# Masked attention and two MLP layers on one core: where q is split, how maxima are taken, the mask's place in a score tile, and single x operations per head

## What is computed

```python
scores = scale * np.matmul(q, k.transpose(0, 1, 3, 2))      # scale = 1/8
mask = block_i >= block_j                                   # blocks of 64 tokens
scores = np.where(mask, scores, -1000000000.0)
scores = scores - np.max(scores, axis=-1, keepdims=True)
attn = np.exp(scores)
attn = attn / (np.sum(attn, axis=-1, keepdims=True) + 1e-09)
attn_out = np.matmul(attn, v)
x = attn_out.transpose(0, 2, 1, 3).reshape(2304, 512)
h = x @ w_in;  x = (h * np.clip(h + 3.0, 0.0, 6.0) / 6.0) @ w_out      # first layer, 512 -> 2048 -> 512
h = x @ w_in2; out = (h * np.tanh(softplus(h))) @ w_out2               # second layer
```

## Time and profile before

| | |
|---|---|
| median of 3 runs | 995.29 us (994.14 to 995.41) |
| the profiled execution's own time | 994.92 us |
| its span | 993.1 us |
| PE busy | 963.6 us, 97% of the span |
| DVE busy | 759.8 us, 77% |
| ACT busy | 648.4 us, 65% |
| POOL busy | 464.0 us, 47%, all of it in the first 512 us |
| granted TensorE clock | 1.00 throughout |

### The profile page before, as it was taken

One profiled execution on the slowest core, in us unless ns is written; L12 is line 12 of the kernel. 1 busy time (PEld: TensorE's weight loads), 2 busy tenths in 40 slices (PEclk: granted clock), 3 DMA queues, 4 the chain that ended last, 5 costly groups with the idle time before them and its releaser, 6 DMA issues.

```text
span 993.1 us, 17891 instructions
## 1 busy us (share of the span) xinstructions
PE 963.6 (97%) x6132; PEld 858.2 (86%) x6132; DVE 759.8 (77%) x1283; ACT 648.4 (65%) x1429; POOL 464.0 (47%) x441
## 2 busy tenths in 40 slices
PE   6999999999999999999999999999999999999998
PEld 5887888899888888998889999899899898998996
DVE  5998888878686866879797786876877877776654
ACT  6888888856555554544445556777777777776663
POOL 7888899967676576968686680000000000000000
PEclk9999999999999999999999999999999999999999
DMA  6778867564689978587977545546645645465255
GB/s 160 211 189 228 222 167 200 151 172 147 221 286 318 321 257 288 182 290 274 316 245 256 199 153 188 222 158 229 219 170 205 230 178 194 170 232 195 93 186 197
DMA packets 81914, 211.49 MB, mean 213 GB/s; under 512 B 12320, under 2 KB 19104, under 8 KB 81824
## 3 DMA queue, kind: packets, MB, share of 16 engines
q1 hardware_dynamic: 81744, 210.06, 65.0%
q10 hardware_dynamic: 80, 0.29, 0.1%
HBM read 170.39 MB, written 39.92 MB: 212 GB/s over the span
## 4 chain that ended last, share of the span: by engine, by line
PE 87%; DVE 7%; issue 3%; ACT 2%; DMA 1%; POOL 1%; SPq 0%; ACTq 0%; DVEq 0%; POOLq 0%
PE psum L956 36%; PE psum L839 11%; PE psum L840 11%; PE psum L841 11%; PE psum L789 5%; PE psum L768 5%; PE psum L744 3%; PE psum L749 3%; DVE ebuf L1519 1%; DVE glo L1525 1%; DMA ext_d<-ext_made 1%; DVE wlo L1417 1%; PE psum L747 1%; DVE ext_made L1425 1%; DMA qkin<-in_qk 1%
## 5 line engine op out<-in xcount | busy, mean ns | idle before, releaser
L956 PE MATMUL psum<-ghi,osplit 128*128 128x512 f32 (+1 forms) x640 | 215.3, 370 | 0.3 <-POOL osplit L1770 0.3
L839 PE MATMUL psum<-xhi,whi 128*128 128x256 f32 (+1 forms) x640 | 187.6, 293 | 2.0 <-ACT snap L1166 2.0
L841 PE MATMUL psum<-xhi,wlo 128*128 128x256 f32 (+1 forms) x640 | 187.5, 293 | 0.0
L840 PE MATMUL psum<-xlo,whi 128*128 128x256 f32 (+1 forms) x640 | 187.4, 293 | 0.0
L956 PE MATMUL psum<-osplit,ghi 128*128 128x512 f32 x576 | 181.2, 396 | 1.4 <-DVE glo L1525 1.4
L1525 DVE SCALAR_TENSOR_TENSOR glo<-ebuf,ghi 128x512 fp32r<-128x512 f32 x144 | 129.9, 902 | 22.5 <-ACT ghi L1214 14.2
L839 PEld LDWEIGHTS psum<-xhi,whi 128*128 128x128 f32 x640 | 121.4, 190 | 15.0 <-ACT snap L1166 3.2
L1770 POOL TENSOR_TENSOR osplit<-oraw,osplit 128x512 fp32r<-128x512 f32 x80 | 117.5, 1471 | 35.7 <-ACT osplit L1133 31.7
L956 PEld LDWEIGHTS psum<-ghi,osplit 128*128 128x128 f32 x640 | 118.1, 189 | 15.8 <-issue 0.4
L840 PEld LDWEIGHTS psum<-xlo,whi 128*128 128x128 f32 x640 | 121.2, 189 | 10.1
L1214 ACT ACTIVATE ghi<-ebuf 128x512 fp32r<-128x512 f32 x144 | 90.1, 626 | 59.4 <-DVE ebuf L1519 37.4
(11 more groups left out here) (113 smaller groups left out, 2252.2 us busy)
## 6 DMA issues: line engine op xcount, KB each, us to landing
ext<-ext_d SPq DMA_DIRECT2D x56, 768.0 KB, 4.4
osplit<-o_d SPq DMA_DIRECT2D x80, 512.0 KB, 5.2
oraw<-in_w_out SPq DMA_DIRECT2D x80, 256.0 KB, 5.8
qkin<-in_qk SPq DMA_DIRECT2D x63, 288.0 KB, 4.3
wraw<-in_w_in SPq DMA_DIRECT2D x32, 512.0 KB, 5.3
ext_d<-ext_made SPq DMA_DIRECT2D x32, 384.0 KB, 5.8
attn_t<-ostage SPq DMA_DIRECT2D x64, 144.0 KB, 3.1
o_d<-staged SPq DMA_DIRECT2D x32, 256.0 KB, 5.4
```

Source lines behind the costliest of these rows:

```text
L839: pe.matmul(dst, hi, xh, start=(start and cc == 0), stop=False, skip_group_check=True)
L840: pe.matmul(dst, hi, xl, start=False, stop=False, skip_group_check=True)
L841: last = pe.matmul(dst, lo, xh, start=False, stop=(stop and cc == 1), skip_group_check=True)
L956: last = pe.matmul(bank(Y_BANK + c, n), stat, mov, start=(first and m == 0), stop=(final and m == 2), skip_group_check=True)
```

## The change

Five edits, all in attention.

1. q is no longer scaled. ScalarE writes `qs` high directly (`split_q_hi`, now L1024), for all heads; GpSimd's cast of q (L1648) is gone. Since `qs` of head n+1 must be free, ScalarE now waits for the scores of head n+1, and the operation stands before the exponential of tile 3 instead of behind that of tile 0.
2. The factor 1/8 goes into the exponential's scale and into the maximum. The maximum is now a `tensor_scalar` (times -1/8) that writes the scaled tile into `prob`, with an accumulator output by minimum into `negmax`.
3. The mask is float32r and is the first matmul of a tile (start=True); `khi` follows. The constants are made with two more GpSimd casts at the start.
4. GpSimd's order: `khi`, v low, x, `klo`, `qs` low.
5. x of the first block: the addition in steps 12, 14, 16 and 18, the multiplication in steps 13, 15, 17 and 19, the rest one step earlier; its four loads go in pairs in steps 9 and 10.

```diff
-EARLY_X_LOAD, NEXT_X_LOAD = (9, 10, 11, 12), (27, 29)
-EARLY_X_ADD, EARLY_X_MIX, EARLY_X_HI, EARLY_X_LO = (14, 16, 18, 20), 21, (22, 23, 24), (23, 24, 25)
+EARLY_X_LOAD, NEXT_X_LOAD = {9: (0, 1), 10: (2, 3)}, (27, 29)
+EARLY_X_ADD, EARLY_X_SCALE, EARLY_X_MIX = (12, 14, 16, 18), (13, 15, 17, 19), 20
+EARLY_X_HI, EARLY_X_LO = (21, 22, 23), (22, 23, 24)
...
-        mask_rows = sb("mask_rows", [P, P], BF16)
-        mask_val = sb("mask_val", [P, DH], BF16)
-        negmax = [sb(f"negmax{s}", [P, NT], F32) for s in range(2)]
+        mask_rows = sb("mask_rows", [P, P], F32R)
+        mask_val = sb("mask_val", [P, DH], F32R)
...
                 for pb, k0, w in pieces:
-                    pe.matmul(bank(pb, w), q_tile, khi[s][:, k0:k0 + w], start=True, stop=False)
                     if i < 4:
-
                         pe.matmul(bank(pb, DH, PW[i] - DH), mask_rows[:, :], mask_val[:, :],
-                                  start=False, stop=False, skip_group_check=True)
-                    last = pe.matmul(bank(pb, w), q_tile, klo[s][:, k0:k0 + w], start=False, stop=True)
+                                  start=True, stop=False, skip_group_check=True)
+                    pe.matmul(bank(pb, w), q_tile, khi[s][:, k0:k0 + w], start=(i == 4), stop=False,
+                              skip_group_check=True)
+                    last = pe.matmul(bank(pb, w), q_tile, klo[s][:, k0:k0 + w], start=False, stop=True,
+                                     skip_group_check=True)
...
-            def scale_q(n):
+            def split_q_hi(n):
 
                 act.wait_ge(qk_loaded[n % QK], 32 * (n // QK + 1))
-                q = qkin[n % QK][:, 0, :]
-                if n == 0:
-                    nc.scalar.activation(qs[0][:, 0:SEQ], q, ACT.Copy, scale=SCALE).then_inc(first_q_hi, 1)
-                else:
-                    nc.scalar.activation(q, q, ACT.Copy, scale=SCALE).then_inc(q_scaled, 1)
+                if n >= 2:
+                    act.wait_ge(scores_ready, ST * (n - 1))
+                nc.scalar.activation(qs[n % 2][:, 0:SEQ], qkin[n % QK][:, 0, :], ACT.Copy).then_inc(q_hi, 1)
...
-                nc.scalar.activation(dst, src, ACT.Exp, bias=negmax[s][:, i:i + 1],
+                nc.scalar.activation(dst, src, ACT.Exp, bias=negmax[s][:, i:i + 1], scale=SCALE,
                                      accum_out=rowsum[n // HEADS % 2][:, col:col + 1]).then_inc(exp_done, 1)
...
-                dve.wait_ge(first_q_hi, 1)
-                nc.vector.scalar_tensor_tensor(out=low, in0=qkin[0][DH:P, 0, :], scalar=SCALE, in1=low.bitcast(F32),
-                                               op0=ALU.mult, op1=ALU.subtract).then_inc(first_q_lo, 1)
+                dve.wait_ge(q_hi, 1)
+                nc.vector.tensor_tensor(low, qkin[0][DH:P, 0, :], low.bitcast(F32), ALU.subtract).then_inc(first_q_lo, 1)
 
             def row_max(n, i):
...
-                    nc.vector.reduce_max(negmax[s][:, i:i + 1], bank(b, PW[i]), AX.X, negate=True
-                                         ).then_inc(max_ready, 1)
...
+                if i == 0 and n >= 2:
+                    dve.wait_ge(p_transposed, PT * (n - 1))
+                src, dst = score_tile(n, i)
+                nc.vector.tensor_scalar(dst, src, -SCALE, None, ALU.mult, ALU.min,
+                                        accum_out=negmax[s][:, i:i + 1]).then_inc(max_ready, 1)
...
-            def split_q_hi(n):
-                s = n % 2
-                pool.wait_ge(q_scaled, n)
-                if n >= 2:
-                    pool.wait_ge(scores_ready, ST * (n - 1))
-                nc.gpsimd.tensor_copy(qs[s][:, 0:SEQ], qkin[n % QK][:, 0, :]).then_inc(q_hi, 1)
-
...
+            def scale_x(blk, k):
...
                 pool.wait_ge(x_added, DC * blk + k + 1)
                 nc.gpsimd.tensor_tensor(x[:, 0, :], x[:, 0, :], x[:, 2, :], ALU.mult).then_inc(x_scaled, 1)
...
+            raw_rows, raw_val = oraw[0][:, 0:P], oraw[0][:, P:P + DH]
+            nc.gpsimd.memset(raw_rows, 0.0).then_inc(memset_done, 1)
+            nc.gpsimd.memset(raw_val, MASKED).then_inc(memset_done, 1)
...
+            nc.gpsimd.tensor_copy(mask_val[:, :], raw_val).then_inc(consts_ready, 1)
+            pool.wait_ge(memset_done, 6)
+            nc.gpsimd.tensor_copy(mask_rows[:, :], raw_rows).then_inc(consts_ready, 1)
```

More of the change, by code:

```diff
@@ L9 @@
 F32R = mybir.dt.float32r
-BF16 = mybir.dt.bfloat16
 AX = mybir.AxisListType
@@ L251, in build @@
         ebuf = [[sb(f"ebuf{s}{f}", [P, TB], F32) for f in range(2)] for s in range(2)]
-        three = sb("three", [P, 1], F32)
-        one = sb("one", [P, 1], F32)
+        small = sb("small", [P, 2 + 2 * NT], F32)
+        three, one = small[:, 0:1], small[:, 1:2]
+        negmax = [small[:, 2 + s * NT:2 + (s + 1) * NT] for s in range(2)]
         ident = sb("ident", [P, P], F32)
-        mask_rows = sb("mask_rows", [P, P], BF16)
-        mask_val = sb("mask_val", [P, DH], BF16)
-        negmax = [sb(f"negmax{s}", [P, NT], F32) for s in range(2)]
+        mask_rows = sb("mask_rows", [P, P], F32R)
+        mask_val = sb("mask_val", [P, DH], F32R)
         rowsum = [sb(f"rowsum{s}", [P, P], F32) for s in range(2)]
@@ L452, in score_banks, with score_tile @@
             return (own + other + (own[0],))[i]
+        def score_tile(n, i):
+            s, b = n % 2, score_banks(n, i)
+            if i < 4:
+                return bank(b, PW[i]), prob[s][:, POFF[i]:POFF[i] + PW[i]]
+            return (bank(b, 2 * BANK).rearrange("p (a k) -> p a k", a=2)[:, :, 0:SEQ // 2],
+                    prob[s][:, POFF[4]:POFF[4] + SEQ].rearrange("p (a k) -> p a k", a=2))
         def pt_done(n, u):
@@ L669, in _ @@
                     load_w(EARLY_LOADS[n])
-                if n in EARLY_X_LOAD:
-                    c = EARLY_X_LOAD.index(n)
+                for c in EARLY_X_LOAD.get(n, ()):
                     if c == 0:
@@ L1052, in attention_step @@
                 if in_use(n + 3) and n < -1:
-                    scale_q(n + 3)
+                    split_q_hi(n + 3)
                 if in_use(n + 1):
                     exps(n + 1, 0)
-                if in_use(n + 3) and n >= 0:
-                    scale_q(n + 3)
                 if in_use(n + 1):
@@ L1065, in attention_step @@
                     split_probs_hi(n, 2)
+                if in_use(n + 3) and n >= -1:
+                    split_q_hi(n + 3)
                 if in_use(n + 1):
                     exps(n + 1, 3)
-                if n == -1:
-                    scale_q(n + 3)
                 if n in EARLY_X_HI:
@@ L1697, in attention_step @@
                     split_k_hi(n + 3)
-                    split_q_hi(n + 3)
-                    split_q_lo(n + 3)
                 if in_use(n + 1):
                     split_v_lo(n + 1)
-                if in_use(n + 3) and n + 3 > 0:
-                    split_k_lo(n + 3)
                 if n in EARLY_X_ADD:
                     add_x(0, EARLY_X_ADD.index(n))
+                if n in EARLY_X_SCALE:
+                    scale_x(0, EARLY_X_SCALE.index(n))
                 if n == EARLY_X_MIX:
@@ L1709, in attention_step @@
                     split_x_lo(0, 0, EARLY_X_LO.index(n))
+                if in_use(n + 3) and n + 3 > 0:
+                    split_k_lo(n + 3)
+                    split_q_lo(n + 3)
                 if n == LAST:
@@ L1713, in attention_step @@
                     add_x(1, 0)
+                    scale_x(1, 0)
                     add_x(1, 1)
+                    scale_x(1, 1)
                     mix_x(1, 0)
@@ L1726, in add_x @@
                 nc.gpsimd.tensor_tensor(x[:, 0, :], x[:, 0, :], x[:, 1, :], ALU.add).then_inc(x_added, 1)
+            def scale_x(blk, k):
+                if KIND[blk] == SHORT:
+                    x = xst_plain[:, k, :, :]
+                else:
+                    x = x_staged(blk, k // 2, k % 2)
                 pool.wait_ge(x_added, DC * blk + k + 1)
@@ L1782, in next_x @@
                         add_x(blk, part + 2 * cc)
+                        scale_x(blk, part + 2 * cc)
                     if t == -6 and part == 0:
@@ L1812, in _ @@
                     add_x(1, 3)
+                    scale_x(1, 3)
                     mix_x(1, 1)
```

34 lines of the change are left out of this document (10 added, 24 removed).

## The result

The changed kernel takes 1000.43 us (median of 5 runs, 999.73 to 1003.17) against 995.29 (median of 5, 994.14 to 996.24) for the kernel before: a ratio of **1.0061 [1.0043, 1.0080]**. It is slower by 5 us where 4 us less were forecast. The profiled execution took 1003.17 us with a span of 1001.4, the slowest of its five runs, so its stretches add up to +8.3 against the span before of 993.1; the last sections say which part of that no median shows.

What follows compares the result with a forecast made beforehand. TensorE bounds free steps, GpSimd x steps. Free steps +1.3, x steps -3.7, MLP-weight steps -1.6, start -0.3, last step about 0.1 less: -4.4, rounded to -4, from 995.3 to 991.3 us; range 988 to 996.

Steps and rivals of the forecast that it cites:

- What bounds the kernel: Before the change: TensorE bounds free attention steps at 5.755 us, GpSimd the twelve x steps at 6.39 each.
- q on ScalarE: Moved q delays tile 3's exponential; tile 1 starts at 2.56 instead of 2.04, cover 0.14; free steps become 5.94 us.
- first rival: The new TensorE wait is not there; VectorE sets the step at 5.65 us; 985 us; chance 0.16.
- The mask: Float32r mask as a tile's first matmul: a pass takes 0.11 us, TensorE's work falls by 0.31 to 5.45 a step.
- third rival: The mask's weight load is not hidden: 0.09 us more a masked tile, 0.6 a step, 1007 us; chance 0.04.
- the same sum: Free step in attention: 5.755 - 2.04 + 2.56 - 0.34 for tiles 1 to 3, giving 5.94 us.
- x steps: Twelve steps with x: GpSimd falls to 5.4, under 5.94; the stretch takes 72.9 us, 3.7 less.
- fourth rival: The relief does nothing: x steps stay at GpSimd's pace since q's low part waits for ScalarE; 995 us; chance 0.07.
- Steps that split an MLP weight: Eleven steps at 5.94 us plus 0.84 in each of four with `wlo`, 0.7 for others: 69.4, 1.6 less.
- VectorE: Five maxima a step each gain an accumulator read of 0.09 us; VectorE reaches 5.65, which the 5.94 step covers.
- second rival: VectorE becomes the bound, with 0.20 us a read and steps of 6.3; 1001 us; chance 0.15.
- Start: Ahead of head 0: VectorE's first split of q takes 1.0 to 1.84 us without its multiplication; 0.3 less.

Runs made afterwards that it cites:

- e5: The changed kernel with q back in its old slot from head 3 on, x loads one a step and x work two steps later: 988.55 us, ratio 0.9917.
- e8: e5 with the mask matmul left out of the computation: 984.64 us, one run.
- e9: The kernel before with only the scaling of q moved ahead of the exponential of tile 3: 1001.47 us, ratio 1.0064.
- e6: The changed kernel with x loads one a step and all work on x two steps later: 1000.74 us, ratio 1.0040.
- e2: The changed kernel with q directly behind the exponential of tile 3 instead of ahead of it: 991.91 us, ratio 0.9963.
- e12: The kernel before with the mask edit alone, small tiles merged so later addresses move, second timing: 994.26 us, ratio 0.9979.
- e1: The changed kernel with q back between the exponentials of tiles 0 and 1 from head 3 on: 993.73 us, ratio 0.9980.

## Why the prediction was wrong

**What bounds the kernel: right.** Free steps were TensorE's, and x steps GpSimd's. e5 and e8 show it: free steps are back at 5.75 with q out of the way and fall to 5.40 when TensorE has less to do; x steps fall when GpSimd has less.

**q on ScalarE: right, in mechanism and size.** I took from the order that the exponential of tile 3 stands behind q, that TensorE waits for it, and that the cover is 0.14: tile 1 at 2.56. It came at 2.63. e9 shows the mechanism alone, with 2.52; the first rival, that the wait isn't there, falls.

**The mask: this is the step that failed.** The prediction has "A mask of 64 columns therefore costs 0.20, 0.31 and 0.25 us in tiles 1 to 3" and "TensorE's own work falls by 0.31 to 5.45 a step". It fell by 0.01. I had worked out two passes from their columns, subtracted them from the masked tile, and booked all that was left to the mask. The yardstick, passes of 288 columns in 0.13 each, was read off a tile's third and fourth pass; its first takes 0.21 (25.69 to 25.90 in the changed kernel) for the same columns. So what a tile's first pass takes more (0.34 for 512 columns in e8, 0.22 by the yardstick) was booked to the mask, and in tile 2 what the last one takes more (0.27 for 384 columns against 0.17). e8 shows the tiles without a mask, and with them a mask of 0.11 to 0.13 in either type. The new mask pass was forecast well, 0.11 against 0.11 to 0.13; the old one was priced too high. The text held the warning, "At 0.19 it would fall by nothing", but took only the new price as uncertain, not the old one.

The 0.15 of "issue" ahead of the bfloat16 load misled me: the load starts late, and is over 0.10 later. The float32r load takes 0.19, and the tiles come out the same. What the Trainium skill (TensorE: Matmul & The Clock Gate, section on weight-path perf modes) states, that bfloat16 weights are read faster and FP32 gains nothing, agrees with the rows of the loads (0.10 before, 0.19 after). The price that the third rival made of it, 0.09 more a masked tile, did not come.

With the mask at nothing the same sum gives 5.755 - 2.04 + 2.56 = 6.275 instead of 5.94, 0.335 more in some 27 steps, 9 us. From -4 that is +5, which is what was measured. That the two agree to the microsecond is partly luck, since the sum has no term for the addresses: in e6's profile, with no late load and no fall of the clock, attention is 6.1 longer than before (221.5 against 215.3) and the MLP layers are 2.8 shorter. One term of the sum turned its sign; this case was in none of my rivals, since the third one had the mask slower than before, and the second got the right time by another mechanism.

**x steps: right relief, wrong step beneath it.** 12 x 5.94 = 71.3 became 12 x 6.33 = 76.0, hardly less than the 76.6 before. GpSimd's own 5.44 a step (65.33 over twelve) is about the 5.4 forecast, but lies under the new wait. The fourth rival has the stretch right, 76.5 against 76.6, and the reason wrong: GpSimd no longer sets these steps.

**Steps that split an MLP weight: wrong for the same reason, and the cover was partly there.** Four of the eleven have `wlo` in the chain; they take 7.38, 7.50, 7.45 and, in e6, where no x load is late, 7.38, against 7.12, 6.98, 7.01 and 6.89. The other seven stood at 5.75 to 6.33 before and take 6.32 to 6.51. That is +3.2 for the stretch without the late load (8.80 in the change's profile against 7.38 in e6: 1.4 more), where -1.6 was forecast. The mask's 0.335 in eleven steps is 3.7 of these 4.8. Most of the rest lies in the four steps with `wlo`: with the mask put right they should take 6.275 + 0.84 = 7.12, so less of `wlo` hid in the new wait than the 0.5 that I had taken.

**VectorE: right that it is covered, too high in size.** 0.09 a read was 0.00: the next operation starts with the read. By the prediction's own numbers VectorE would have passed 5.94 at 0.15 a read ((5.94 - 5.2) / 5), not at 0.17. The second rival, VectorE as the bound at 1001 us, came out at nearly the measured time, and is false: that time was reached with VectorE idle for 0.85 of a free step. That a read instruction of its own exists, as the Trainium skill says (VectorE: DVE Perf Modes, section on two Vector instructions with no wait between them), the trace now shows, 0.08 long. A right number doesn't carry its reason.

**Start: wrong, small.** VectorE's first split of q, now without the multiplication, took 1.84 as before (the upper bound). VectorE, in order of time:

```profile
6.44 1.84 DVE L1329 TENSOR_TENSOR qs<-qkin,qs 64x576 fp32r<-64x576 f32 x1 [0.26 <-ACT qs L1024]
```

The +1.5 there has another source, for the most part the clock (below): without its fall head 0 stands at 21.17 in e2, 21.32 in e5 and 21.76 in e6, though at 22.25 in e12, whose clock did not fall either. With the late x load this makes the profiled execution the slowest of its five. Against e6's, the same but for x and 4.9 us shorter, head 0 is 1.1 later, steps 12 and 13 take 8.80 and 7.19 instead of 7.38 and 6.34, and the MLP layers the remaining 1.4.

**Not tried.** The wait for the scores wasn't taken out by itself in the changed kernel: `qs` is read by those scores. What is known is e9, where q in the same place has no such wait, and e1, where the wait is long over.

## What to carry to other kernels

An operation in an in-order queue costs what stands behind it: the same 0.57 us of ScalarE were free between two exponentials that were early, and 0.5 us a step ahead of the one that TensorE waits for. To price an instruction that is to be changed, don't subtract a computed rest from a measured whole: find, or run, the same place without the instruction, and treat the old price as uncertain as the new one. When a median moves and no step does, suspect what the edit did on the side, here the addresses, and run that alone.
